# Two stacked feed-forward layers on one core: six seven-product pairs per tile of layer 1, and its output summed in DRAM by adding transfers

## The reference

```
a = softmax(normalised k transposed @ normalised q / tau)      # 256 x 256
x = v @ a                                                      # 6016 x 256
h = x @ w_in1;  g = where(h > 0, h, exp(min(h, 0)) - 1)
x = g @ w_out1                                                 # y of layer 1, 6016 x 256
h = x @ w_in2;  g = h / (1 + exp(-h))
out = g @ w_out2                                               # 6016 x 256
```

## Time and profile before

| | |
|---|---|
| three runs | 1001.96, 1002.33, 1002.90 us; median 1002.33 us |
| the profiled execution, its own time | 1002.03 us |
| its span, first to last instruction | 1000.2 us |
| granted TensorE clock, mean | 1.000 |
| PE busy | 994.1 us, 99% of the span |
| DVE, ACT busy | 852.1 us (85%), 738.3 us (74%) |
| POOL busy | 10.2 us |

### The profile page before, as it was taken

The page is one execution under the profiler, slowest core; times in us unless marked ns, Lnnn a source line. Parts: engine busy times, 40 slices in busy tenths (PEclk is TensorE's granted clock), DMA queues, the critical chain, the costliest instruction groups (busy, mean ns, idle before and its releaser), DMA issues.

```text
span 1000.2 us, 14653 instructions
## 1 busy us (share of the span) xinstructions
PE 994.1 (99%) x5256; PEld 898.1 (90%) x5256; DVE 852.1 (85%) x1046; ACT 738.3 (74%) x1125; POOL 10.2 (1%) x11
## 2 busy tenths in 40 slices
PE   9999999999999999999999999999999999999998
PEld 8888999899999998999999888888888888888997
DVE  7779899999999999998896777887888888888886
ACT  6789888888888888888886666666666666666664
POOL 0300000000000000000000000000000000000000
PEclk9999999999999999999999999999999999999999
DMA  9913212312213123030003433344335235234333
GB/s 349 377 21 74 43 50 41 90 48 44 69 22 90 48 43 88 37 83 22 1 20 148 135 111 115 112 102 166 105 81 194 73 94 178 100 94 131 111 101 89
DMA packets 137404, 97.54 MB, mean 98 GB/s; under 512 B 114176, under 2 KB 120832, under 8 KB 137344
## 3 DMA queue, kind: packets, MB, share of 16 engines
q1 hardware_dynamic: 136736, 96.26, 32.1%
q10 hardware_dynamic: 608, 0.49, 0.2%
HBM read 77.07 MB, written 19.66 MB: 97 GB/s over the span
## 4 chain that ended last, share of the span: by engine, by line
PE 98%; DMA 0%; DVE 0%; issue 0%; ACT 0%; DVEq 0%
PE banks L1366 50%; PE banks L1571 21%; PE banks L1509 13%; PE banks L1481 10%; PE banks L1376 4%; DMA early_qk<-k 0%; PE banks L1605 0%; PE banks L1478 0%; PE banks L1613 0%; DVE m_tile L1345 0%; PE banks L1409 0%; DVE out_tile L1356 0%; PE banks L1415 0%; ACT early_scores L737 0%; DVE early_scores L1007 0%
## 5 line engine op out<-in xcount | busy, mean ns | idle before, releaser
L1366 PE MATMUL banks<-x_parts,w_in_parts 128*128 128x512 f32 (+1 forms) x1152 | 274.9, 375 | 0.0
L1366 PE MATMUL banks<-xT_parts,a_w_in 128*128 128x512 f32 (+1 forms) x1152 | 259.3, 375 | 0.1
L1366 PEld LDWEIGHTS banks<-x_parts,w_in_parts 128*128 128x128 f32 x1152 | 215.6, 189 | 28.5 <-ACT g_pair L887 1.0
L1571 PE MATMUL banks<-g_pair_parts,w_forms 128*128 128x512 f32 (+1 forms) x987 | 239.3, 375 | 0.0
L1366 PEld LDWEIGHTS banks<-xT_parts,a_w_in 128*128 128x128 f32 x1152 | 213.6, 189 | 23.9 <-issue 0.5
L1571 PEld LDWEIGHTS banks<-g_pair_parts,w_forms 128*128 128x128 f32 x987 | 186.5, 189 | 22.1
L887 ACT ACTIVATE g_pair<-banks 128x512 f32<-128x512 f32 (+1 forms) x192 | 112.8, 588 | 126.8 <-PE banks L1366 119.7
L1049 DVE SCALAR_TENSOR_TENSOR g_raw<-g_raw,banks 128x1024 f32<-128x1024 f32 (+1 forms) x96 | 114.9, 1197 | 26.5 <-ACT g_raw L776 24.8
L1251 DVE TENSOR_TENSOR g_pair_parts<-g_forms,g_pair_parts 128x1024 fp32r<-128x1024 f32 (+1 forms) x96 | 115.1, 1200 | 21.8 <-ACT g_pair_parts L896 21.6
L896 ACT ACTIVATE g_pair_parts<-g_forms 128x1024 fp32r<-128x1024 f32 (+1 forms) x96 | 99.4, 1036 | 33.9 <-PE banks L1571 33.3
L776 ACT ACTIVATE g_raw<-g_raw 128x512 f32<-128x512 f32 (+1 forms) x192 | 119.5, 622 | 5.8
(11 more groups left out here) (112 smaller groups left out, 864.7 us busy)
## 6 DMA issues: line engine op xcount, KB each, us to landing
w_forms<-w_forms SPq DMA_DIRECT2D x48, 896.0 KB, 4.6
w_forms<-w_out_forms SPq DMA_DIRECT2D x8, 896.0 KB, 4.2
early_qk<-q SPq DMA_DIRECT2D x23, 256.0 KB, 7.4
early_qk<-k SPq DMA_DIRECT2D x22, 256.0 KB, 7.8
y_raw<-y_sums SPq DMA_DIRECT2D x40, 128.0 KB, 2.1
x_parts<-y_raw SPq DMA_DIRECT2D x10, 512.0 KB, 5.7
out<-out_tile SPq DMA_DIRECT2D x40, 128.0 KB, 2.7
v_in<-v SPq DMA_DIRECT2D x36, 128.0 KB, 3.5
```

The source lines that it names most:

```text
L1366: mm = pe.matmul(dst, lhsT, rhs, start=first and n == 0, stop=last and n == len(todo) - 1)
L1571: mm = pe.matmul(m_banks[m][:, 0:u.n], ring[k % N_RING][:, form, x, :], by_turns(gp2[k % 2][:, y, operand, 0:u.n]), start=k == 0 and part ...
```

## The change

1. **One more seven-product pair.** `ONE_WINO` becomes (0, 1, 2, 3, 4, 5), in tiles 1 to 11. Its weight forms need space: the five later ones stay in `forms1`, those of pair 0 go to a new place in the second half of the `x_parts` buffer (`forms10`), made by four more sums, one high part and one low part in tile 0 (`one_forms_sum` 4 to 7, slots 4 and 5; hi in slot 6; lo in slot 7). The `w_out2` forms get one buffer instead of two.
2. **No sums on DVE.** `y_sum_u2`, `y_sum_u3` and `y_row` go. ACT copies each of the four banks to SBUF as it is: bank 4 in slot 0 and bank 5 in slot 1 of the next tile (`one_copy`, twice), and banks 6 and 7 in slot 1 (`row_copy`, twice), 128 x 512 each. The copies of tile t wait until all adding transfers of tile t - 1 are done (`d_add`), since they reuse the buffer.
3. **Sums in DRAM.** `spill` stores M1 to all four blocks of the tile (one transfer, 512 KB, SP). POOL then issues four transfers with an add, each after the one before it has landed: M6 to three blocks (384 KB), M5 to two (256 KB), M7 to two (256 KB), and the four plain parts to four (512 KB). A block is 128 x 256 float32, 128 KB.
4. **Layout.** `y1_raw` is kept in blocks, so `x_load` becomes four transfers of 128 KB with runs of 256 bytes in SBUF in place of one; the spill has runs of 1 KB.
5. **Moved.** `v_transpose` goes from the end of DVE's slot 1 to the start of slot 0, and `vT_hi` from slot 2 to slot 0. `relu` waits only for the plain low parts of the pair two slots back where that is a seven-product pair, no longer for its sums.
6. At the join to layer 2, ACT copies banks 4 and 5 between the first `silu`s, banks 6 and 7 in slot 2; ACT, DVE and SP wait for the last adding transfers later in the first tile of layer 2.

The core of the diff:

```diff
-SLOTS_LEAD = 0, 2
+SLOTS_LEAD = 0,
-SLOT_V_TURN, SLOT_V_HI, SLOT_V_LO = 1, 2, 6
-SLOT_FIRST_Y, SLOT_ROWS = 2, 1
-SLOT_COPY, SLOT_SUM_U2, SLOT_SUM_U3 = 7, 7, 0
+SLOT_V_TURN, SLOT_V_HI, SLOT_V_LO = 0, 0, 6
+SLOTS_M_COPY, SLOT_ROWS = (0, 1), 1
-ONE_WINO = (0, 2, 3, 4, 5)
-BLOCKS_OF_PAIR = (0, 5, 1, 2, 3, 4, 6, 7)
+ONE_WINO = (0, 1, 2, 3, 4, 5)
+BLOCKS_OF_PAIR = (7, 0, 1, 2, 3, 4, 5, 6)
...
@@ sync, spill
                 if t == 0:
-                    sp.wait_ge(y0_copy, CB)
+                    sp.wait_ge(y_rows, CB)
+                    src = y_part(ONE[0], Y_C22, 4).rearrange("p (s x) -> p s x", s=4)
                 else:
-                    sp.wait_ge(c1_sum, Y_SUMS * t)
-                for c in range(CB):
-                    for h in range(2):
-                        dst = y1_raw[t * P:(t + 1) * P, c, 0:n].rearrange("p (m h b) -> p m h b", m=4, h=2)
-                        sp.dma_start(dst[:, :, h, :], y_raw(ONE[t], c)[:, h, :, :]).then_inc(d_spill, 16)
+                    sp.wait_ge(d_spill, 16 * t)
+                    sp.wait_ge(m1_copy, 2 * t - 1)
+                    src = y_part(ONE[t], Y_M1).rearrange("p (s x) -> p s x", s=1).broadcast_to([P, 4, n // 2])
+                sp.dma_start(y1_blocks(t, n), src).then_inc(d_spill, 16)
@@ gpsimd
+            def add_to_y1(ph, step, blocks, src):
+
+                if step:
+                    pool.wait_ge(d_add, 16 * (N_ADDED * (ph.tile - 1) + step))
+                pool.dma_start(y1_blocks(ph.tile, ph.n)[:, blocks, :], src, accum_op=ALU.add).then_inc(d_add, 16)
+
+            for ph in ONE[1:]:
+                part = lambda slot, n: y_part(ph, slot).rearrange("p (s x) -> p s x", s=1).broadcast_to([P, n, ph.n // 2])
+                pool.wait_ge(d_spill, 16 * ph.tile + 16)
+                pool.wait_ge(m1_copy, 2 * ph.tile)
+                add_to_y1(ph, 0, slice(Y_C22, Y_C12 + 1), part(Y_M6, 3))
+                add_to_y1(ph, 1, slice(Y_C22, Y_C12 + 1, 2), part(Y_M5, 2))
+                add_to_y1(ph, 2, slice(Y_C22, Y_C21 + 1), part(Y_M7, 2))
+                pool.wait_ge(y_rows, 2 * ph.tile + 2)
+                add_to_y1(ph, 3, slice(Y_C22, Y_C11 + 1), y_part(ph, Y_C22, 4).rearrange("p (s x) -> p s x", s=4))
@@ scalar
-                if one_pair(ph, k) >= 2:
-                    act.wait_ge(u_lo, 2 * one_pair(ph, k) - 2)
+                two_before = shifted(ph, k, 2, PAIRS)
+                if two_before:
+                    act.wait_ge(u_lo, 2 * one_pair(*two_before) + (1 if two_before[1] in two_before[0].wino else 2))
...
                 act.wait_ge(p1_down, one_pair(ph, ph.wino[-1]) + 1)
-                act.wait_ge(d_spill, N_SPILLS * 16 * ph.tile)
-                act.activation(y_sum(ph, slice(Y_P1, Y_P5 + 1, Y_P5 - Y_P1)).rearrange("p s (m b) -> p s m b", m=4),
-                               bank[4][:, 0:ph.n].rearrange("p (s b m) -> p s m b", s=2, m=4), ACT.Copy).then_inc(m1_copy, 1)
+                if ph.tile > 1:
+                    act.wait_ge(d_add, 16 * N_ADDED * (ph.tile - 1))
+                act.activation(y_part(ph, (Y_M1, Y_M7)[i], 2).rearrange("p (s m b) -> p s m b", s=2, m=4),
+                               bank[4 + i][:, 0:ph.n].rearrange("p (s b m) -> p s m b", s=2, m=4), ACT.Copy).then_inc(m1_copy, 1)
@@ tensor, wino_down
                         if b >= 6:
                             rows_free(ph, b - 6)
-                        elif ph.tile > 1 and b == 4:
-                            pe.wait_ge(m1_copy, ph.tile - 1)
                         elif ph.tile > 1:
-                            pe.wait_ge(c1_sum, Y_SUMS * (ph.tile - 2) + 2)
+                            pe.wait_ge(m1_copy, 2 * (ph.tile - 2) + b - 3)
```

More of the change, by code:

```diff
@@ L155, in build @@
         at_ysum = cursor[0]
[L156 removed]
+        ysum = place("y1_parts", [P, 8 * T // 2], F32)
         at_end = at_ysum + 2 * WP * 4
@@ L370, in build, with y_part, y1_blocks @@
         in_two = lambda x: x.rearrange("p (a j) -> p a j", a=2)
[L372 to L382, removed]
+        def y_part(ph, first, n=1):
+            return ysum[:, first * ph.n // 2:(first + n) * ph.n // 2]
+        def y1_blocks(t, n):
+            return y1_raw[t * P:(t + 1) * P, :, 0:n // 2]
         def next_x(u):
@@ L638, in _ @@
             ring_load(0, 1)
+            spill(NT - 1, T_LAST)
             sp.wait_ge(p1_down, NT * PAIRS)
@@ L807, in first_y_copy @@
-            def first_y_copy(ph):
-                act.wait_ge(w_split, n_split(IN2 + N_PIECES - 1))
-                for c in range(CB):
-                    if c == 0:
-                        act.wait_ge(y_done, 1)
-                    else:
-                        act.wait_ge(p1_down, PAIRS)
-                    act.activation(y_raw(ph, c), y_banks[c][:, 0:ph.n].rearrange("p (h b m) -> p h m b", h=2, m=4),
-                                   ACT.Copy).then_inc(y0_copy, 1)
+                if ph.tile > 1:
+                    act.wait_ge(d_add, 16 * N_ADDED * (ph.tile - 1))
@@ L844, in slot_one @@
                 is_wino = back is not None and back[1] in back[0].wino
-                if ph.tile == 1 and k == SLOT_FIRST_Y:
-                    first_y_copy(ONE[0])
+                for i in range(2):
+                    if ph.tile > 1 and k == SLOTS_M_COPY[i]:
+                        one_copy(ph.before, i)
                 lead = ph.tile == 0 or ph.tile == 1 and k in SLOTS_LEAD
@@ L860, in slot_one @@
                     one_sums_hi(*back)
-                if ph.wino and k == SLOT_COPY:
-                    one_copy(ph)
+                for c in range(CB):
+                    if ph.before and k == SLOT_ROWS:
+                        row_copy(ph.before, c)
                 if ph.v_next and k == (SLOT_V_HI if ph.tile else SLOT_ZERO_V_HI):
@@ L919, in tile @@
                         normal_hi(ONE[-1], PAIRS - 1)
+                    if u is TWO[0] and k == PAIRS - 1:
+                        act.wait_ge(d_add, 16 * N_ADDED * (NT - 1))
                     for i in range(4):
@@ L1180, in slot_one @@
                 back = shifted(ph, k, 1, PAIRS)
-                if ph.tile > 1 and k == SLOT_SUM_U3:
-                    y_sum_u3(ph.before)
+                if ph.tile and ph.v_next and k == SLOT_V_TURN:
+                    v_transpose(*ph.v_next[:2])
                 lead = ph.tile == 0 or ph.tile == 1 and k in SLOTS_LEAD
@@ L1187, in slot_one @@
                     v_transpose(*ph.v_next[:2])
-                for n in range(4):
+                for n in range(8):
                     if ph.tile == 0 and k == SLOTS_ONE_FORMS_SUM[n]:
@@ L1200, in slot_one @@
                     normal_lo(*back)
-                if ph.wino and k == SLOT_SUM_U2:
-                    y_sum_u2(ph)
-                for c in range(CB):
-                    if ph.tile > 1 and k == SLOT_ROWS:
-                        y_row(ph.before, c)
                 if weights_in_slot(ph, k) is not None:
                     weights_lo(dve, weights_in_slot(ph, k))
-                if ph.tile and ph.v_next and k == SLOT_V_TURN:
-                    v_transpose(*ph.v_next[:2])
                 for c in range(CB):
@@ L1326, in tile @@
                         plain_lo(*back)
-                    for c in range(CB):
-                        if u is TWO[0] and k == 1:
-                            y_row(ONE[-1], c)
             tiles_two(dve, tile)
```

182 lines of the change are left out of this document (96 added, 86 removed).

## The result

The changed kernel takes **1008.88 us** (median of 4 runs, 1008.61 to 1009.36), the kernel before 1002.15 in the same series: ratio 1.0066, 95% interval 1.0049 to 1.0084. Forecast were 1000.3 us and a range up to 1003.5.

A forecast was written before the change was run, and what follows sets the result against it. PE, busy 99% of the span, was taken as the bound. Seven-product savings of 2.22 us less 0.14 (short tiles) and 0.05 (stall) gave about 2.0 us off the median 1002.33: 1000.3 us, range 999.5 to 1003.5.

The forecast's parts named there:

- "Cost 0" for SP and layer 2: Spill, loads and the eight x_load transfers per layer 2 tile fit into existing slack, so they cost 0.
- PE's work: Layer 1: a seven-product pair saves 0.247 us in tiles 1 to 9, costs 0.14 together in 10 and 11; net 2.08 us.
- The floor of 111 ns a matmul: Short tiles 10 and 11: 21 matmuls of 224 columns take as long as with 256, some 111 ns each.
- Rival 4: Short matmuls go by columns after all: tiles 10 and 11 gain 0.22 us each, 999.7 us; chance 2%.
- DVE 37.84 us a tile: Layer 1: DVE stays at some 37.6 us busy of a 39.97 us tile; ACT rises to 36.4.
- `one_g` of pair 0: Layer 1: it starts at about T0 + 4.1 us, T0 being the start of a tile's first `up`; before, T0 + 4.92.
- rival 2: ACT or DVE come late in the row of six seven-product slots: 0.3 us a tile, +3.3 us, 1003.6; chance 8%.
- Tile 1: Stall where PE's seven products of pair 0 want DVE's last part: 0.05 us, bounds 0 and 0.6.
- Rival 3: POOL's issuing of four transfers a tile holds DVE up: +2.4 us in each of 10 tiles, 1024 us; chance 4%.
- The chain of additions: Four adding transfers a tile, begun at T0 + 5.8, take 11 to 58 us, nearest row 31; room 35.7; no stall.

The follow-up runs named there:

- e2: The changed kernel with 58 more wait instructions in PE's stream of layer 1: 1000.37 us, ratio 0.9979 to the kernel before.
- e5: The kernel before with 198 more instructions in PE's stream of layer 1 (five waits at each of 66 places): 1010.64 us, ratio 1.0086.
- e8: The changed kernel with pair 1 again done with plain products, so only y's way through DRAM is new: 1007.82 us, ratio 1.0054 to the kernel before.
- e9: e8 with 20 more instructions in ACT's stream of layer 1: 1002.82 us, ratio 1.0006 to the kernel before.
- e11: The kernel of e2 with the additions to y in eight transfers a tile instead of four, same bytes: 1006.13 us, ratio 1.0040 to the kernel before.

## Why the prediction was wrong

**The step that failed** is "Cost 0" for SP and layer 2, more exactly the belief behind it that layer 2's engines do the same as before because none of their lines is changed. The sum had no term for the place of layer 2's loop in an engine's instruction stream. That term is +8.5 us (changed kernel less e2). In the profiled execution 5.0 us of it are standing still and 2.9 us are work at half clock; the remaining 0.6 us I can't place. e5 shows it in the kernel before, e2 takes it out of the changed one, e8 shows it for ACT. No rival named it. The profile's page had a sign of it, 36 packets on q8, and the diff says that PE's stream grows. The Trainium skill (Runtime: NRT & Kernel Launch, "Instruction fetch mechanics") gives PE room for 128 KiB, filled in blocks of 16 KiB, which makes eight, and says that a taken branch whose target isn't in the current window of two pages has to wait for it. By that room, and taking one piece as fetched ahead, seven pieces of loop just fit and eight don't, as the runs show; the window of two pages, though, does not agree with the kernel before, where PE jumps back six pieces with no fetch. The measurement decides.

**What held**, point by point:

- PE's work: 0.25 us less in each of the tiles from 3 to 9, as forecast, and some 0.07 more in 10 and 11. With the loop in place the measured gain is 1002.46 - 1000.37 = 2.1 us; forecast 2.0. That the two agree to 0.1 us is in part luck: the interval of the gain runs from 1.1 to 3.0 us, and in the traces of the kernel before and of e2 layer 1 gets only about 1.4 us shorter, because of tile 1 (below). The floor of 111 ns a matmul holds with 224 columns: 2.33 us. Rival 4 is out.
- DVE 37.84 us a tile (37.6 forecast), ACT 36.67 (36.4), `one_g` of pair 0 at T0 + 3.9 (4.1). From tile 2 on six seven-product slots in a row stayed in time, so rival 2 is out as a cost in every tile.
- Tile 1 was mis-sized. I took 0.05 us with bounds of 0 and 0.6, at the down of pair 0. The stop comes behind the row of six, ahead of the down of pair 6:

```profile
138.26 1.56 PE L1485 MATMUL banks<-g_parts,w_out_parts 128*128 128x512 f32 x6 [0.42 <-DVE g_parts L1089]
```

  The two tiles 1 and 2 together take 80.8 us and took 80.6 before; two seven-product pairs should have made them 0.5 us shorter, so this term is 0.7 us, over its upper bound. In e9, with pair 1 plain, DVE's low part is late as well, by 1.0 us ahead of the down of pair 1, and the two tiles take 81.7 us: some 0.5 us of the 2.4 above come from there.
- Rival 3: `one_g` takes 1.22 us as before, and DVE's 37.84 us a tile are close to the forecast's, so POOL's issuing did not stretch DVE's work. It is out.
- The chain of additions: forecast were bounds of 11 and 58 us and 31 as the likeliest; it took some 21 us (226.67 to 242.99, and the last landing). What I missed is that it starts later. The transfer that spills the first copy to `y1_raw` has to land ahead of it: issued at 219.40, it landed 7.0 us later, so the first addition goes out at T0 + 10.8 and not at T0 + 5.8. (Over the tiles of 512 rows it goes out between T0 + 5.9 and T0 + 11.5, in most near T0 + 9.) The room in this tile was T0 + 41.5 less T0 + 10.8, 30.7 us and not 35.7, and e11, with 32, shows ACT waiting. The direction of the forecast stood on a margin that was 3 to 5 us smaller in most tiles than I said.

**What stays open.** Why the stop is two gaps of 2.3 and 2.8 us in one layout and one of 6.65 in another; how much of it is the fetch itself; and what makes up the 13 to 16 and the 51 to 70 instructions that my count misses. The numbers of held pieces (eight, and four of 8 KB) are what the runs agree with, one loop each; a loop with another length was not tried. The trace names no releaser for the gaps of PE; that it waits there for its instruction packets is inferred, since the gaps and the new packets come and go together in every run.

## What to carry to other kernels

If a kernel has a loop, its code ahead of the loop is part of the loop's speed: count the instruction packets on the page before and after (q8 and q14 here), and if they grow by more than the stream did (here 46 against the 37 of e2), look at the jump back. Here a few dozen idle instructions moved the body to a better place: the changed kernel with 58 waits beats the kernel before by 0.21% (0.11 to 0.30), the changed one without them loses 0.66%. A timed comparison of two kernels with a loop can therefore measure the luck of the layout; pad both before judging an edit. For a chain of dependent transfers, begin to count at the landing of the one it rests on, and count both their number and their bytes.

## What the runs showed of the hardware that I had not expected

- PE keeps a loop body of 1561 instructions over a jump back without any fetch if it touches seven pieces of 16 KB, and fetches it all again if it touches eight: 46 packets in place of the 37 of e2, 8 us, once. By the counts above, 24 of 256 starting places are bad for this length (232 to 255). For ACT's 311 instructions in pieces of 8 KB it is, by an estimate from the same counts, 54 of 128.
- With the stop of 5.0 us the granted clock fell to 0.50, between its two parts, and stayed there until 772 us; that added 2.9 us, more than half of the stop's own length.
- An addition in DRAM issued by POOL takes 4.8 to 6.6 us for 256 to 384 KB with its issue of 1.1 to 1.3 us, and about 4.0 us for 128 to 256 KB; from issue to landing 512 KB take 5.4 us and 128 KB take 3.2.
- Two waits in a row on an engine may share one instruction: 198 added waits were 132 instructions.
